# Preparing the next round's tokens on VectorE and ScalarE in place of GpSimd, with new places for the down sums

## What is computed

```python
def reference(...):                       # batch 8, heads 8, seq 576, head_dim 64, 32 packed queries
    attn_out = _attn_ref(**attn_kwargs)   # p attends to k, v; q attends to the result
    x = attn_out as (4608 tokens, 512)
    x = _moe_ref(x=x, ...)                # rms norm; silu(xn @ w_gate) * (xn @ w_val) @ w_out, d_ff 1536
    return _moe2_ref(x=x, ...)

def _moe2_ref(x, w_in, w_out, alpha):     # d_model 512, d_ff 2048
    h = x @ w_in
    g = np.maximum(h, 0.0) + alpha * np.minimum(h, 0.0)
    return (g @ w_out).astype(np.float32)
```

## Time and profile before

| | us |
|---|---|
| median of 3 runs (lowest, highest) | 1556.11 (1551.54, 1559.9) |
| the profiled execution | 1560.53 |
| its span, first to last instruction | 1558.7 |
| TensorE busy, mean granted clock | 1478.5 (95%), 0.982 |
| VectorE busy | 1070.6 (69%) |
| ScalarE busy | 691.7 (44%) |
| GpSimd busy | 444.3 (29%) |

### The profile page before, as it was taken

One profiled execution on the slowest core, in us unless ns is written; L12 is line 12 of the kernel. 1 busy time (PEld: TensorE's weight loads), 2 busy tenths in 40 slices (PEclk: granted clock), 3 DMA queues, 4 the chain that ended last, 5 costly groups with the idle time before them and its releaser, 6 DMA issues.

```text
span 1558.7 us, 23935 instructions
## 1 busy us (share of the span) xinstructions
PE 1478.5 (95%) x9334; PEld 1254.2 (80%) x9334; DVE 1070.6 (69%) x1496; ACT 691.7 (44%) x1141; POOL 444.3 (29%) x379
## 2 busy tenths in 40 slices
PE   8999999999999999999998799979997899789998
PEld 5988778777878788798887688868886788678887
DVE  6675757566565757524368966896679857985686
ACT  4554544534444544422355235622563346333553
POOL 2704224343313234325003700181007300640000
PEclk9999999999999999999999899989999999989999
DMA  9315675858586673562366376736664576547664
GB/s 358 104 41 178 196 237 155 275 155 258 173 240 215 177 241 95 169 222 85 122 200 253 117 236 216 260 133 188 225 242 162 187 227 212 206 144 239 210 216 155
DMA packets 167152, 301.07 MB, mean 193 GB/s; under 512 B 21760, under 2 KB 121088, under 8 KB 152576
## 3 DMA queue, kind: packets, MB, share of 16 engines
q1 hardware_dynamic: 166896, 299.48, 59.5%
q10 hardware_dynamic: 144, 0.07, 0.0%
HBM read 244.59 MB, written 54.92 MB: 192 GB/s over the span
## 4 chain that ended last, share of the span: by engine, by line
PE 79%; DVE 17%; ACT 2%; DMA 1%; issue 1%; SPq 0%; POOL 0%; ACTq 0%; DVEq 0%; POOLq 0%
PE psum L904 25%; PE psum L906 24%; PE psum L905 24%; DVE stage_lo L1950 9%; PE psum L1102 3%; DVE g_sb L1961 2%; DVE e L1672 1%; DVE h_lo L1883 1%; DVE g_sb L1964 1%; DMA rest_mid<-act_sb 1%; PE psum L927 1%; DVE max L1668 1%; DVE an_lo L1773 1%; PE psum L976 0%; DVE act_sb L1879 0%
## 5 line engine op out<-in xcount | busy, mean ns | idle before, releaser
L904 PE MATMUL psum<-stage_hi,ring 128*128 128x462 f32 (+1 forms) x560 | 222.9, 398 | 54.6 <-DVE stage_lo L1950 54.4
L1950 DVE TENSOR_TENSOR stage_lo<-g_sb,stage_hi 128x462 fp32r<-128x462 f32 (+1 forms) x240 | 245.6, 1052 | 29.5 <-ACT stage_hi L1531 28.6
L1531 ACT CAST stage_hi<-g_sb 128x462 fp32r<-128x462 f32 (+1 forms) x240 | 138.8, 578 | 238.8 <-PE psum L906 238.6
L904 PE MATMUL psum<-an_hi,m_hi 128*128 128x288 f32 x768 | 233.4, 304 | 5.5 <-DVE act_sb L1879 3.4
L905 PE MATMUL psum<-an_hi,m_lo 128*128 128x288 f32 x768 | 225.9, 294 | 0.0
L906 PE MATMUL psum<-an_lo,m_hi 128*128 128x288 f32 x768 | 225.7, 294 | 0.0
L906 PE MATMUL psum<-stage_lo,ring 128*128 128x462 f32 (+1 forms) x560 | 217.3, 388 | 0.0
L905 PE MATMUL psum<-stage_hi,ring 128*128 128x462 f32 (+1 forms) x560 | 216.8, 387 | 0.0
L904 PE MATMUL psum<-x_hi,ring 128*128 128x462 f32 (+1 forms) x560 | 209.7, 374 | 0.0
L906 PE MATMUL psum<-x_lo,ring 128*128 128x462 f32 (+1 forms) x560 | 209.0, 373 | 0.0
L905 PE MATMUL psum<-x_hi,ring 128*128 128x462 f32 (+1 forms) x560 | 208.1, 372 | 0.0
(11 more groups left out here) (180 smaller groups left out, 2627.3 us busy)
## 6 DMA issues: line engine op xcount, KB each, us to landing
ring<-w_down SPq DMA_DIRECT2D x70, 1024.0 KB, 5.0
ring<-w_up SPq DMA_DIRECT2D x40, 1024.0 KB, 5.1
gv_sb<-w_gv SPq DMA_DIRECT2D x39, 1024.0 KB, 5.8
ring<-w_up SPq DMA_DIRECT2D x40, 768.0 KB, 4.5
k_sb<-k_t SPq DMA_DIRECT2D x16, 576.0 KB, 5.2
q_sb<-q_t SPq DMA_DIRECT2D x8, 1152.0 KB, 5.5
x_raw<-y_mid SPq DMA_DIRECT2D x16, 462.0 KB, 6.7
w_up<-parts_hi SPq DMA_DIRECT2D x16, 448.0 KB, 6.5
```

Of the source, the lines that this page charges most:

```text
L904: nc.tensor.matmul(dst, w_hi, hi, start=start, stop=False, skip_group_check=onto)
L1531: nc.scalar.copy(stage_hi[:, n % STAGES, 0:w], raw_of(i, j, w)).then_inc(stage_hi_done, 1)
L1950: nc.vector.tensor_tensor(stage_lo[:, n % STAGES, 0:w], raw_of(DOWN_ORDER[p], j, w), stage_hi[:, n % STAGES, 0:w].bitcast(F32), ALU.subtra ...
```

## The change

Four blocks of the next round's x are loaded in the up stage, behind page 6, into the output buffers out_r, out_e, out_h and out_f, which are idle then. VectorE makes the four differences in place there (change_x: x1, x3, x2, x4 behind c21 of columns 1, 2, 4 and 6); three of the four t1 go to columns 3, 5 and 7. Behind page 19 four transfers within SBUF move the differences to x_raw, and behind page 21 blocks 0, 4 and 5 are loaded. The split stands beside the down units: x_hi on ScalarE (X_HI_AFTER), x_lo on VectorE (X_LO_AFTER). The down products go to pairs of banks over all eight, three of them added onto a pair that holds an earlier product (DOWN_ONTO), and the sums are five on VectorE and three copies on ScalarE; no instruction of GpSimd is left in the rounds. GpSimd's cast and subtraction in combine are cut into pieces of 256 elements, and the x work before the first round (same operations as before) into quarters.

```diff
+DOWN_BANKS = [4, 6, 0, 6, 2, 0, 4]
+DOWN_ONTO = [3, 5, 6]
+X_ORDER = [2, 3, 1, 6, 0, 4, 5]
+X_HI_AFTER = [11, 17, 23, 28, 39, 45, 48]
+X_LO_AFTER = [14, 20, 26, 31, 42, 49, 51]
 UNITS = PRODUCTS * DUOS
 UNIT_SLOTS, STAGES = 4, 4
...
         def pair_ps(p, w):
-            return psum[:, 4 + 2 * (p % 2):6 + 2 * (p % 2), 0:w]
+            return psum[:, DOWN_BANKS[p]:DOWN_BANKS[p] + 2, 0:w]
...
+        def x_arrival(i, t):
+            group = {2: 0, 3: 0, 1: 1, 6: 1, 0: 2, 4: 2, 5: 2}[i]
+            return x_in[group], 16 * (2, 2, 3)[group] * t
...
+            def load_blocks_of_x(t):
+
+
+                for name, dst, rows, cols in (("r", out_r, 0, 0), ("e", out_e, 0, 1), ("h", out_h, 1, 1), ("f", out_f, 1, 0)):
+                    reached(sp, o_stored[name], 16 * (t - 1))
+                    sp.dma_start(dst[:, :, 0:WIDTHS[t]], block_of_y(t, rows, cols)).then_inc(x_blocks_in, 16)
+
+            def move_changed_x(t):
+                sp.wait_ge(x_changed, 4 * t)
+                for i, src in ((2, out_r), (3, out_e), (1, out_h), (6, out_f)):
+                    sp.dma_start(x_raw[:, i, :, 0:WIDTHS[t]], src[:, :, 0:WIDTHS[t]]).then_inc(x_arrival(i, t)[0], 16)
+
             def load_x(t):
-                w, at = WIDTHS[t], STARTS[t]
-                for slot, rows, cols in ((0, 0, 0), (2, 0, 1), (4, 2, 0), (5, 2, 1)):
-                    sp.dma_start(x_raw[:, slot, :, 0:w],
-                                 y_mid[:, rows:rows + 2, at + cols * w:at + (cols + 1) * w]).then_inc(x_in, 16)
+                for i, rows, cols in ((0, 0, 0), (4, 1, 0), (5, 1, 1)):
+                    sp.dma_start(x_raw[:, i, :, 0:WIDTHS[t]], block_of_y(t, rows, cols)).then_inc(x_arrival(i, t)[0], 16)
...
                 for n in range(PAGES):
                     if PAGES * t + n >= UNIT_SLOTS:
                         load_page(t, n)
+                    if t > 0 and n == 0:
+                        store_out(t - 1, "h", out_h, 2, 1, o22_done)
                     if t > 0 and n == 1:
-                        store_out(t - 1, "f", out_f, 2, 1, o22_done)
-                    if t > 0 and n == 3:
                         store_out(t - 1, "e", out_e, 0, 1, o12_done)
-                    if t > 0 and n == 5:
-                        store_out(t - 1, "h", out_h, 2, 0, o21_done)
-                    if n == 2 * DUOS + UNIT_SLOTS and t + 1 < ROUNDS:
+                    if t > 0 and n == 4:
+                        store_out(t - 1, "f", out_f, 2, 0, o21_done)
+                    if n == 6 and t + 1 < ROUNDS:
+                        sp.wait_ge(y_stored, 32 * NT)
+                        load_blocks_of_x(t + 1)
+                    if n == 2 * DUOS + UNIT_SLOTS - 1 and t + 1 < ROUNDS:
                         sp.wait_ge(up_mm, PRODUCTS * DUOS * (t + 1))
-                        sp.wait_ge(y_stored, 32 * NT)
+                        move_changed_x(t + 1)
+                    if n == 2 * DUOS + UNIT_SLOTS + 1 and t + 1 < ROUNDS:
                         load_x(t + 1)
-                    if n == 2 * DUOS + 13:
+                    if n == 2 * DUOS + 12:
                         store_out(t, "r", out_r, 0, 0, o11_done)
...
-                nc.gpsimd.tensor_copy(hi[:], raw[:]).then_inc(part_step, 1)
+                for i in range(0, PRODUCTS, 2):
+                    some = slice(i, min(i + 2, PRODUCTS))
+                    copied = nc.gpsimd.tensor_copy(hi[:, some], raw[:, some])
+                copied.then_inc(part_step, 1)
                 pool.wait_ge(part_step, done + 5)
-                nc.gpsimd.tensor_tensor(lo[:], raw[:], hi[:].bitcast(F32), ALU.subtract).then_inc(part_ready, 1)
+                for i in range(0, PRODUCTS, 2):
+                    some = slice(i, min(i + 2, PRODUCTS))
+                    rest_of = nc.gpsimd.tensor_tensor(lo[:, some], raw[:, some], hi[:, some].bitcast(F32), ALU.subtract)
...
+            def quarters(w):
+                return [(k, slice(a * w // 2, (a + 1) * w // 2)) for k in range(2) for a in range(2)]
...
-                        if j == 0:
-                            pe.wait_ge(x_ready, PRODUCTS * t + i + 1)
+                        if j == 0 and t == 0:
+                            pe.wait_ge(first_x_ready, i + 1)
+                        if j == 0 and t > 0 and i == 0:
+                            pe.wait_ge(x_lo_done, PRODUCTS * t)
+                            pe.wait_ge(o12_done, t)
+                            pe.wait_ge(du_done, t)
...
+                if p == 0 and t > 0:
+                    pe.wait_ge(o21_done, t)
+                if p == 1 and t > 0:
+                    pe.wait_ge(o11_done, t)
+                if p == 2:
+                    pe.wait_ge(c11_copied, DUOS * (t + 1))
+                    pe.wait_ge(u_done, DUOS * (t + 1))
+                if p == 3:
+                    pe.wait_ge(d1_copied, t + 1)
+                if p == 4:
+                    pe.wait_ge(c12_done, DUOS * (t + 1))
+                    pe.wait_ge(c21_done, DUOS * (t + 1))
+                if p == 5:
+                    pe.wait_ge(d75_done, t + 1)
+                if p == 6:
                     pe.wait_ge(d7_copied, t + 1)
...
-                                              stage_lo[:, u % STAGES, 0:w], j == 0, j == DUOS - 1)
+                                              stage_lo[:, u % STAGES, 0:w], j == 0 and p not in DOWN_ONTO,
+                                              j == DUOS - 1, p in DOWN_ONTO)
...
             def copy_d7(t):
                 w = WIDTHS[t]
                 act.wait_ge(unit_mm, UNITS * t + DUOS)
-                if t > 0:
+                if t + 1 < ROUNDS:
+                    act.wait_ge(*x_arrival(1, t + 1))
+                else:
                     act.wait_ge(o_stored["h"], 16 * t)
-                nc.scalar.copy(out_h[:, :, 0:w], pair_ps(PRODUCTS * t, w)).then_inc(d7_copied, 1)
...
+            def copy_o11(t):
+                w = WIDTHS[t]
+                act.wait_ge(unit_mm, UNITS * t + 4 * DUOS)
+                if t + 1 < ROUNDS:
...
+            def x_hi_of(t, i):
+                w = WIDTHS[t]
+                act.wait_ge(*x_arrival(i, t))
+                nc.scalar.copy(x_hi[:, i, :, 0:w], x_raw[:, i, :, 0:w]).then_inc(x_hi_done, 1)
...
+                    if t + 1 < ROUNDS and u in X_HI_AFTER:
+                        x_hi_of(t + 1, X_ORDER[X_HI_AFTER.index(u)])
...
+                if name == "c22_half":
...
+                    nc.vector.tensor_tensor(h, h, pair_ps(2, w), ALU.add).then_inc(d75_done, 1)
+                if name == "u":
...
+                    nc.vector.tensor_tensor(r, r, pair_ps(4, w), ALU.add).then_inc(du_done, 1)
...
+                    nc.vector.tensor_tensor(h, h, r, ALU.add).then_inc(o22_done, 1)
...
+                    nc.vector.tensor_tensor(e, r, pair_ps(5, w), ALU.add).then_inc(o12_done, 1)
...
+                    nc.vector.tensor_tensor(f, r, pair_ps(6, w), ALU.add).then_inc(o21_done, 1)
...
+            def change_x(t, name):
+                w, done = WIDTHS[t], 4 * (t - 1)
+                b11, b12, b22, b21 = (x[:, :, 0:w] for x in (out_r, out_e, out_h, out_f))
+                if name == "x1":
+                    dve.wait_ge(x_blocks_in, 16 * 4 * t)
+                    nc.vector.tensor_tensor(b11, b12, b11, ALU.subtract).then_inc(x_changed, 1)
...
+            def x_lo_of(t, n):
+                w, i = WIDTHS[t], X_ORDER[n]
+                dve.wait_ge(x_hi_done, PRODUCTS * (t - 1) + n + 1)
+                nc.vector.tensor_tensor(x_lo[:, i, :, 0:w], x_raw[:, i, :, 0:w], x_hi[:, i, :, 0:w].bitcast(F32),
+                                        ALU.subtract).then_inc(x_lo_done, 1)
+
+            AFTER_C21 = {1: "x1", 2: "x3", 3: "t1 0", 4: "x2", 5: "t1 1", 6: "x4", 7: "t1 2"}
+            BESIDE_UNITS = {7: ["t1 3"], 18: ["t2 0"], 20: ["t2 1"], 23: ["t2 2"], 25: ["t2 3"], 28: ["c22_half"],
+                            34: ["t4 0"], 36: ["t4 1"], 38: ["t4 2"], 40: ["t4 3"], 44: ["u"], 45: ["o22"], 52: ["o12"]}
...
+                    name = AFTER_C21.get(j, "")
+                    if name[:1] == "t":
+                        difference(t, int(name[-1]), name[:2])
+                    if name[:1] == "x" and t + 1 < ROUNDS:
+                        change_x(t + 1, name)
...
+                    if t + 1 < ROUNDS and u in X_LO_AFTER:
+                        x_lo_of(t + 1, X_LO_AFTER.index(u))
```

More of the change, by code:

```diff
@@ L429, in build @@
         ow_in = [sem(f"ow_in{n}") for n in range(len(OW_PIECES))]
-        x_in, x_step, x_ready = sem("x_in"), sem("x_step"), sem("x_ready")
+        first_x_in, x_step, first_x_ready = sem("first_x_in"), sem("x_step"), sem("first_x_ready")
+        x_blocks_in = sem("x_blocks_in")
+        x_in = [sem(f"x_in{n}") for n in range(3)]
+        x_changed, x_hi_done, x_lo_done = sem("x_changed"), sem("x_hi_done"), sem("x_lo_done")
         y_stored = sem("y_stored")
@@ L640, in move_parts, with block_of_y, load_first_x @@
                             load_part(n + PART_SLOTS)
```

(43 more changed lines are left out.)

100 lines of the change are left out of this document (37 added, 63 removed), and 3 rows, old and new, of the table BESIDE_UNITS.

## The result

The changed kernel takes 1469.61 us (median of 4 runs, 1467.44 to 1471.16), the kernel before 1555.57 beside it. The ratio is 0.9446, with a 95% interval of 0.9418 to 0.9474: 86 us less. The forecast was 1477, with a range of 1464 to 1498. The profiled execution took 1469.25 us, its span is 1467.5.

The account below looks back on a forecast made before the run. It took four down stages to be held up by VectorE's late stage_lo beside GpSimd instructions. 1560.5 - 87.2 - 0.5 + 12 - 8 = 1476.8, forecast 1477 us, range 1464 to 1498.

Parts of the forecast that it names:

- GpSimd leaves the down stages: Four down stages that prepare a next round fall from 371.6 us to 4 x 71.1: -87.2 us.
- The last stage: The last round's down stage loses the 0.5 us in which its TensorE is idle: -0.5 us.
- New down work of VectorE and ScalarE, moves of x, down sums: Down stages: added instructions, moves inside SBUF and eight-bank sums are covered by stages held ahead; price 0.
- x1's wait: Up stages: x1 waits for its block load, delaying TensorE's product 5 of column 2; 3.0 us in four rounds, +12.
- the clock, taken as 0: Up stages: the lone new gap of about 3 us brings no slow clock afterwards; 0 us.
- Smaller GpSimd instructions in the first part: First half: combine's GpSimd work cut in four shortens TensorE's seven waits for h_lo; -8 us, between 0 and -11.
- Blocks in time: Rival: up-stage block loads land early enough, so the +12 goes; 1465 us, chance 0.12.
- the clock answers the new gap: Rival: each up-stage gap brings a half-speed stretch, 4 x 1.7 = 7 us more; 1484 us, chance 0.12.
- GpSimd not the cause: Rival: VectorE is slow in down stages by its own queue's load and keeps half the loss; 1520 us, chance 0.03.
- moves too slow: Rival: down stages wait for SBUF moves of x, 2.3 us a round, 9 in all; 1486 us, chance 0.13.
- slower than before: Rival: copy_d7 on ScalarE waits for x1 and x4 in x_raw, delaying later stage_hi; beyond 1560 us, chance 0.02.
- the case that got 0.58: The forecast itself, all terms as priced: 1477 us, chance 0.58.

Follow-up runs that it names:

- e1_slots: Changed kernel with VectorE's up-stage slots moved by a column, x1 after c21 of column 2 instead of 1, two t1 beside down units: 1453.04 us, ratio 0.932.
- e7: Kernel before with its x work on GpSimd cut into quarters of 231 elements in all rounds, nothing else changed: 1536.92 us, ratio 0.9868.
- e3: Kernel before with only combine's cast and subtraction on GpSimd cut into pieces of 256 elements: 1542.12 us, ratio 0.9891.
- e4: Changed kernel with combine's cast and subtraction on GpSimd whole again, 896 elements: 1487.58 us, ratio 0.9541.
- e2_page5: Changed kernel with the four block loads behind page 5 instead of page 6, slots unchanged: 1452.91 us, ratio 0.932.
- e11: Changed kernel with x work of rounds 1 to 4 back on GpSimd in quarters, TensorE's first up products each waiting for their own x_lo: 1467.4 us, ratio 0.9415.
- e9: Changed kernel plus 40 useless GpSimd copies of 832 elements in each of the first four down stages: 1543.31 us, ratio 0.9907.
- e8_x_back: Changed kernel with x work of rounds 1 to 4 back on GpSimd in whole instructions, the rest of the change kept: 1530.82 us, ratio 0.9831.
- e5: Changed kernel plus 20 useless GpSimd multiplications of 832 elements in each of the first four down stages: 1559.41 us, ratio 1.0016.
- e6: Changed kernel plus 60 useless GpSimd memsets of 832 elements in each of the first four down stages: 1469.53 us, ratio 0.9435.

## Why the prediction was right, and where its sizes were not

- **GpSimd leaves the down stages, -87.2.** Right in mechanism and size: 371.6 to 284.4 by the stages. Useless multiplications bring the whole loss back, memsets do not.
- **The last stage, -0.5.** Measured -0.7.
- **New down work of VectorE and ScalarE, moves of x, down sums: 0.** Right: no wait of TensorE in any down stage, ScalarE never waits for x_raw. The last of the moves is issued at 814.31, 3.0 us into the stage, and lands after 8.3 us, at 11.3, and at 11.5 to 11.7 in the other three stages; the forecast said 10.0 to 11.4. copy_d7, which must wait for it, started at 11.7 (823.04). So this price of 0 held by 0.4 us or less, and in e1_slots ScalarE once waited 0.2 us.
- **x1's wait, +12.** Right in mechanism, place and order of events; measured +16.7 (301.1 less 4 x 71.1). The term has two parts. The wait was well sized: x1 waited 23.2 us in four (5.8 each, forecast 5 to 6), TensorE's four gaps for product 5 cost 11.3, and c22 with what else follows a gap 0.5 each, as in the first round, so 13.3 against 12. What was missing is **the clock, taken as 0** on one lone gap. That step failed in two ways. The gap after 869.02 was not lone: it was the third in some 18 us, and the two before it, of 2.79 and 2.20 us of waiting, were each followed by half clock (table of stages, before):

```profile
857.30:860.60 3.30, 3.18 (x9) 2.27 (x8) 3.30 (x2) 0.58 (x1) 3.22 (x3) 0.50 0.10 20
864.10:867.40 3.30, 3.30 (x10) 2.85 (x9) 3.30 (x2) 0.58 (x1) 3.22 (x3) 0.50 0.00 0
```

  And in the changed kernel three of the four gaps were followed by a stretch at 0.50:

```profile
909.80:913.20 3.40, 3.12 (x8) 2.75 (x9) 3.36 (x5) 0.00 (x0) 0.00 (x0) 0.50 0.13 53
```
```profile
1056.50:1060.00 3.50, 3.50 (x11) 3.00 (x10) 3.47 (x5) 0.55 (x1) 0.00 (x0) 0.51 0.22 91
...
1203.30:1206.70 3.40, 3.40 (x11) 2.92 (x10) 3.32 (x5) 0.60 (x1) 0.00 (x0) 0.50 0.11 43
```

  The stage without it is 3.1 us over 71.1, those with it 4.0, 4.5 and 5.1. Less each one's own gap, the three with the slow stretch took 1.1 to 1.3 us more: 3.4 in all. So the rival "the clock answers the new gap", given 0.12, came true in three rounds of four, at somewhat under its price of 1.7. The Trainium skill, TensorE: Matmul & The Clock Gate, section HAM oscillation, which was weighed there, says of gaps that recur that the stretch after each one starts slow; three of the four new gaps agree, the first does not.
- **Smaller GpSimd instructions in the first part, -8 (0 to -11).** Right in mechanism, undersized, and outside its own bounds: measured -20.0 in the trace, of which combine has 16 to 18 by the two runs that change only it. The x work in quarters may have the rest: with it alone (e7) the rounds start at 755.0, 2.1 earlier, little more than the 736.6 to 739.2 over which the versions with both cuts scatter. The step that failed is the counting. I took the seven waits for h_lo alone, and left them half of a piece each. But TensorE's idle time over the whole stretch, which the table of stages gives, was 15 us, and after the change it is 0.2:

```profile
27.50:737.10 709.60, 709.39 (x5706) 597.60 (x5707) 411.36 (x762) 326.03 (x596) 311.59 (x525) 1.00 0.60 183
```

  Waits for act_sb (3.4 us) had the same cause, an instruction of the same queue held up one step earlier: they go in e3 and are back in e4. That no residue stayed, because what is left of a hold fits under the work that VectorE is ahead, is my reading. TensorE's busy time fell by another 4.7 us for the same matmuls (714.1 to 709.4). This too belongs to combine's pieces: it is 710.0 in e3 and back at 713.4 in e4. Whether the matmuls around a wait took longer or are only recorded so stays open. The last 0.5 us lie before 28 us.
- **Blocks in time.** Did not happen (x1 began 24.1 to 25.2 us into the stage, forecast 24.4), but e2_page5 is that case made by hand. It gives 1453 and not the rival's 1465, by the 12 us more that the first part gave.
- **GpSimd not the cause**, **moves too slow**, **slower than before**: none of their signs is in the profile.

The sum as measured: 1560.5 - 87.2 - 0.7 + 16.7 - 20.0 = 1469.3. Two errors of opposite sign, 5 and 12, left 7.5. That the forecast came so near is partly luck: with only the first put right it would have said 1481.5, with only the second 1465. And what happened was not the case that got 0.58, but the clock's.

## What to carry to other kernels

Find a stage of the same kernel in which the suspected engine is quiet: the last round gave the size of the gain to a tenth of a microsecond. Before work is taken off GpSimd, try to cut its instructions, so short that the held-up instruction still takes less time than the waiting engine needs for a unit of work: 0.92 us on average in e11 against a unit of 1.27. To be shorter than the stock of 2.4 us is not enough, as the copies of e9 show. Cutting, with waits for each operand by itself, was worth 63 of the 78 us between e8_x_back and e1_slots, and 16 to 18 in the first part for a few lines. An instruction that waits for a load goes where the load has certainly landed, since everything behind it in its engine's queue waits too, and a lone gap of TensorE of 3 us should be priced with a slow stretch after it.

## What was not expected of the hardware

- Memsets on GpSimd (795 ns for 832 elements) left VectorE at 637 ns a stage_lo; 40 copies with one input a stage raised its mean to 983, 20 multiplications to 1003. That the means are so near comes from the counts. A held stage_lo took about 1.3 us beside copies and 2.0 beside the longer multiplications: whether GpSimd reads decides that VectorE is held, and the length of its instruction for how long.
- The hold works both ways. The copies of e9 took 883 ns at their shortest and 1295 on average beside VectorE, where the memsets stayed between 791 and 802; the x_lo quarters of e11 took 970 ns in the rounds and 748 before them.
- Four transfers within SBUF of 462 KB landed 1.2 us apart, as loads from DRAM of that size did.
- Five traces have x1's wait at column 1 (the changed kernel, e4, e5, e6, e9), so 20 gaps of TensorE in stages where it is busy otherwise, 2.6 to 4.0 us from the start of one matmul to that of the next. In the second to fourth round all 15 were followed by half clock, one of 2.60 us too. In the first round one of five was (e5, 2.62 us), and not one of 2.84 (e4). So the length of the gap does not decide it here; what does stays open.
